# Expert 0's blocks without a fetch of their sums, the last gate on column groups, value loads issued by ScalarE

## The reference

```python
# attention: 8 heads of 64; heads 0-3 see 32 past positions, heads 4-7 every 4th of 128
attn = softmax(where(mask, q @ k.T / 8, -1e9)) ; x = attn @ v          # -> (2304, 512)
h = x @ w_in ; x = (h * cos(h)) @ w_out                                 # 512 -> 2048 -> 512
noisy = x @ w_gate + log1p(exp(x @ w_noise)) * noise                    # 8 experts
top2, top2_w = the two largest of noisy per token, their softmax
for e in range(8):                                                      # 512 -> 1024 -> 512
    for the rows routed to e: out[row] += weight * (relu(x[row] @ w1[e]) @ w2[e])
```

## Time and profile before

| what | us |
|---|---|
| median of three runs | 1009.43 |
| profiled execution, its own time | 1009.55 |
| its span, first to last instruction | 1007.8 |
| TensorE busy | 992.0 (98%) |
| VectorE busy | 575.2 (57%) |
| ScalarE busy | 445.8 (44%) |
| POOL busy | 354.9 (35%) |
| DMA engines, queue of SP | 22.2% of 16 engines |
| granted TensorE clock | 1.00 |

### The profile page before, as it was taken

One profiled execution on the slowest core, in us unless ns is written; L12 is line 12 of the kernel. 1 busy time (PEld: TensorE's weight loads), 2 busy tenths in 40 slices (PEclk: granted clock), 3 DMA queues, 4 the chain that ended last, 5 costly groups with the idle time before them and its releaser, 6 DMA issues. The chain is left out here.

```text
span 1007.8 us, 17738 instructions
## 1 busy us (share of the span) xinstructions
PE 992.0 (98%) x6176; PEld 877.2 (87%) x6176; DVE 575.2 (57%) x1189; ACT 445.8 (44%) x1091; POOL 354.9 (35%) x349
## 2 busy tenths in 40 slices
PE   7999999999999999999999999999999999999998
PEld 5878898888889889889888888999898989999896
DVE  4888766576576576576676754434344444424322
ACT  5989665453454544534547333333132323323111
POOL 2656786222222222222231355143241425133241
PEclk9999999999999999999999999999999999999999
DMA  9787356000000000005006154434353533434130
GB/s 203 178 177 170 74 138 227 33 2 1 31 1 31 0 1 31 1 0 186 14 12 231 55 187 137 144 108 143 130 176 113 177 130 109 142 125 154 41 110 30
DMA packets 101252, 99.60 MB, mean 99 GB/s; under 512 B 72707, under 2 KB 73187, under 8 KB 101184
## 3 DMA queue, kind: packets, MB, share of 16 engines
q1 hardware_dynamic: 86352, 66.38, 22.2%
q0 software_dynamic: 10000, 31.15, 10.0%
q10 hardware_dynamic: 4832, 1.18, 0.7%
HBM read 80.61 MB, written 20.07 MB: 100 GB/s over the span
## 5 line engine op out<-in xcount | busy, mean ns | idle before, releaser
L1807 POOL TENSOR_TENSOR g_lo<-gate,g_hi 128x384 fp32r<-128x384 f32 x95 | 98.0, 1031 | 278.3 <-ACT g_hi L1099 278.3
L1159 ACT ACTIVATE uh_hi<-ps 128x306 fp32r<-128x306 f32 (+1 forms) x112 | 47.8, 426 | 274.1 <-PE ps L155 270.3
L154 PE MATMUL ps<-ux_lo,w_hi 128*128 128x306 f32 (+1 forms) x448 | 136.5, 305 | 0.0
L155 PE MATMUL ps<-ux_hi,w_hi 128*128 128x306 f32 (+1 forms) x448 | 136.0, 304 | 0.0
L153 PE MATMUL ps<-ux_hi,w_lo 128*128 128x306 f32 (+1 forms) x448 | 135.8, 303 | 0.1
L153 PE MATMUL ps<-x_hi,w_lo 128*128 128x384 f32 x384 | 133.6, 348 | 0.1
L1543 DVE SCALAR_TENSOR_TENSOR uh_lo<-ps,uh_hi 128x306 fp32r<-128x306 f32 (+1 forms) x112 | 53.3, 476 | 136.3 <-ACT uh_hi L1159 127.8
L155 PE MATMUL ps<-x_hi,w_hi 128*128 128x384 f32 x384 | 129.3, 337 | 0.0
L154 PE MATMUL ps<-x_lo,w_hi 128*128 128x384 f32 x384 | 129.2, 337 | 0.0
L153 PE MATMUL ps<-w_hi,g_lo 128*128 128x512 f32 x288 | 114.0, 396 | 0.5 <-DVE g_lo L1504 0.5
L155 PE MATMUL ps<-w_hi,g_hi 128*128 128x512 f32 x288 | 114.0, 396 | 0.0
(11 more groups left out here) (230 smaller groups left out, 2033.3 us busy)
## 6 DMA issues: line engine op xcount, KB each, us to landing
xT<-in_w SPq DMA_DIRECT2D x32, 1024.0 KB, 9.2
out<-table SPq DMA_DIRECT2D x18, 256.0 KB, 3.9
y_rows<-y_sb SPq DMA_DIRECT2D x6, 768.0 KB, 3.5
y_sb<-in_w_out SPq DMA_DIRECT2D x16, 256.0 KB, 3.4
q_raw<-in_q SPq DMA_DIRECT2D x40, 96.0 KB, 3.2
k_raw<-in_k SPq DMA_DIRECT2D x30, 96.0 KB, 2.8
w_raw<-in_w_in SPq DMA_DIRECT2D x4, 512.0 KB, 5.0
v_near<-in_v SPq DMA_DIRECT2D x8, 256.0 KB, 3.7
```

Source lines behind the costliest of these rows:

```text
L154: nc.tensor.matmul(psum, s_hi, m_lo, start=False, stop=False)
L155: return nc.tensor.matmul(psum, s_hi, m_hi, start=False, stop=stop)
L1159: nc.scalar.activation(u_h[0][:, f, piece_at[piece]], psH[:, f % 2, 0:PIECE[piece]], ACT.Relu).then_inc(u_hhi, 1)
L1807: nc.gpsimd.tensor_tensor(g2[1][:, f % 2, :], gate[:, f % 2, :], g2[0][:, f % 2, :], ALU.subtract).then_inc(glo_done, 1)
```

## The change

Four things, which can be read apart from each other.

- `acc`, `gather_acc` and their semaphores are gone. `finish(g)` multiplies alone and waits for the scatter of block g-1 in place of the fetch. The early blocks' scatters take their index from where it lies, without a copy, and the first one waits for the zeroed output.
- The last tile's gate is `gate_all`, `copy_turned`, `turn_back`, `copy_all_logits`, as in the loop. The three transposed blocks have three places.
- At the end of the last tile `first_part(0, 1)` on ScalarE goes behind `g_hi` of chunk 15, and `last_low_g` on VectorE goes ahead of all weight parts, `low_x(0)` ahead of `first_part(0, 1)`.
- `load_v(0, 1)` and `load_v(0, 2)` are issued by ScalarE behind `copy_q(0)` and `copy_q(1)` and their keys; `load_w(1)`, `(2)` and `(3)` by ScalarE at the end of steps 3, 6 and 9.

```diff
@@ tiles
-        acc = at(g2_at + 4 * F2, "acc", [P, DM])
+        behind = xT[:].rearrange("p c s -> p (c s)")[:, QUANTA * QW:]
+        yT_end = yT + [behind[:, 0:DM].rearrange("p (d q) -> p d q", q=P)]
+        turned_end = behind[0:GN, DM:DM + P]
@@ SP
-            load_w(0)
-            load_v(0, 1)
+            load_w(sp, 0)
             load_qk(NT)
-            load_v(0, 2)
             for s in range(NT + 1, STEPS + GROUPS):
...
-                if s in (NT + 2, NT + 5, NT + 8):
-                    load_w((s - NT + 1) // 3)
@@ TensorE, behind the last tile
             first_product(0, (1,))
-            gate_y(LAST, 0, 0)
             transpose_x(1)
-            gate_y(LAST, 1, 1)
+            gate_all(LAST)
             transpose_h(0, (0,))
-            gate_y(LAST, 2, 0)
+            turn_back(LAST)
             transpose_h(0, (1,))
@@ ScalarE, tile
-                    if last and f == FC - 1:
-                        first_part(0, 1)
                     act.wait_ge(g_done, m + 1)
...
                     nc.scalar.activation(g2[0][:, f % 2, :], gate[:, f % 2, :], ACT.Copy).then_inc(ghi_done, 1)
-                    if last and f == FC - 2:
-                        first_part(0, 0)
+                    if last and f >= FC - 2:
+                        first_part(0, f - FC + 2)
@@ ScalarE, attention
                 if s < 2:
                     load_rows(act, NT - 2 + s, k, k_raw)
+                    load_v(act, 0, s + 1)
...
+                if s in (3, 6, 9):
+                    load_w(act, s // 3)
@@ ScalarE, behind the last tile
             relu(0, 0)
-            copy_yT(LAST, 0, yT_last[0], yT[0])
-            copy_yT(LAST, 1, yT_last[1], yT[1])
-            copy_logits(LAST, 0)
-            copy_yT(LAST, 2, yT_last[2], yT[0])
+            for b in range(TB):
+                copy_yT(LAST, b, yT_last[b], yT_end[b])
             relu(0, 1)
-            copy_logits(LAST, 1)
             copy_x(1)
-            copy_logits(LAST, 2)
+            copy_turned(LAST)
+            copy_all_logits(LAST)
@@ VectorE, finish
-                dve.wait_ge(acc_in, 16 * (g + 1))
-                nc.vector.scalar_tensor_tensor(out=res[:], in0=eO, scalar=e_all[:, bass.ds(g, 1)], in1=acc[:],
-                                               op0=ALU.mult, op1=ALU.add).then_inc(res_done, 1)
+                if not (isinstance(g, int) and g == 0):
+                    dve.wait_ge(scattered, 16 * g)
+                nc.vector.tensor_scalar(res[:], eO, e_all[:, bass.ds(g, 1)], None, ALU.mult).then_inc(res_done, 1)
@@ VectorE, behind the last tile
+            last_low_g()
             first_part(0, 0)
-            last_low_g()
+            low_x(0)
             first_part(0, 1)
-            low_x(0)
@@ POOL
+            def scatter(g):
+                to = idx_s
+                if isinstance(g, int):
+                    to = slots(1, g)
+                else:
                     pool.wait_ge(scattered, 16 * g)
+                    nc.gpsimd.tensor_copy(idx_s, slots(1, g)).then_inc(iss, 1)
+                    pool.wait_ge(iss, g + 1)
+                if isinstance(g, int) and g == 0:
+                    pool.wait_ge(out_zero, 16 * NB)
                 pool.wait_ge(res_done, g + 1)
...
             gather_x(1)
-            pool.wait_ge(l2_done, FC * NTT)
-            gather_acc(0)
...
                 if g + 2 != EARLY:
-                    scatter(g - 1, g + 2 > EARLY)
+                    scatter(g - 1)
                 if g + 2 > EARLY:
-                    index_acc(g)
                     unit_gather(0, 1, idx_ua, 1)
-                gather_acc(g, g + 2 > EARLY)
-                if g + 2 > EARLY:
                     unit_gather(0, 2, idx_ua, 2)
...
                 scatter(g - 1)
-                gather_acc(g)
             scatter(last)
```

More of the change, by code:

```diff
@@ L393, in load_rows, with load_v, load_w @@
                 eng.dma_start(to[o:o + n, NH:H, :], dilated(src, b)[r, j:j + n, :, :]).then_inc(signal, 16)
+        def load_v(eng, b, g):
+            if b > 0:
+                eng.wait_ge(pv_done, NT * (b - 1) + g + GROUPS + 1)
+            near, p0 = v[b, 0:NH, :, :].rearrange("h (u s) d -> s (h u) d", u=2), WINDOW if g == 0 else 0
+            eng.dma_start(v_near[p0:P, g, :, :, :].rearrange("p h u d -> p (h u) d"),
+                         near[g * TQ - WINDOW + p0:(g + 1) * TQ]).then_inc(v_in_near[g], 16)
+            if g == 0:
+                eng.dma_start(v_near[0:WINDOW, g, :, 1, :],
+                             v[b, 0:NH, S // 2 - WINDOW:S // 2, :].rearrange("h s d -> s h d")
+                             ).then_inc(v_in_near[g], 16)
+            for t in (g, g + GROUPS):
+                for o, r, j, n in segments(t * TQ - WINDOW, TK):
+                    eng.dma_start(v_dil[o:o + n, t, :, :], dilated(v, b)[r, j:j + n, :, :]
+                                 ).then_inc(v_in_dil[t], 16)
+        def load_w(eng, j):
+            if j >= TB:
+                eng.wait_ge(wlo_done, 2 * (j - TB) + 2)
+            d, cols = w_chunk(2 * j)
+            eng.dma_start(w_raw[:, j % TB], w_in_v[:, d, cols.start:cols.start + 2 * WCH]
+                         ).then_inc(w_loaded[j % TB], 16)
         def w_chunk(n):
@@ L463, in _ @@
             sp.sem_inc(d_stored, 16)
[L465 to L479, removed]
             def load_qk(s):
@@ L485, in load_qk @@
                 load_rows(sp, s, k, k_raw)
[L487 to L493, removed]
             def load_ring(at, src):
@@ L697, in transpose_y @@
                 x.then_inc(tp_done, 1)
[L699 to L705, removed]
             def gate_all(i):
                 pe.wait_ge(tp_evac, TB * (i + 1))
+                y = yT_end if isinstance(i, int) and i == LAST else yT_all
                 for d in range(DC):
                     for b in range(TB):
-                        x = nc.tensor.matmul(ps_turned[GQ * b:GQ * (b + 1), :], wgn[:, d, 0:GQ], yT_all[b][:, d, :],
+                        x = nc.tensor.matmul(ps_turned[GQ * b:GQ * (b + 1), :], wgn[:, d, 0:GQ], y[b][:, d, :],
                                              start=(d == 0), stop=(d == DC - 1), skip_group_check=True)
```

40 lines of the change are left out of this document (10 added, 30 removed).

## The result

| | before | after |
|---|---|---|
| median, the two compared | 1010.52 us (1009.1 to 1013.75, 20 runs) | 1012.35 us (1010.84 to 1016.67, 20 runs) |
| profiled execution | 1009.55, span 1007.8 | 1013.62, span 1011.9 |
| ratio after to before | | 1.0023, 95% interval 1.0014 to 1.0032 |

The change costs 2.3 us (1.4 to 3.2). It was forecast at 1008.4 and at most 1011.0. Of the 3.9 us between 1008.4 and 1012.35, 1.1 is not in the change: the forecast started from 1009.43, the median of three runs, and the median of 20 runs of the same kernel is 1010.52. The rest is the change, forecast at -1.05 us and measured at +2.3 by the ratio (+1.8 by the two medians). The profiled execution of after is one of its longer ones, so the two profiles stand 4.1 us apart and not 2.3; the traces are used for where the time is, the ratios for how much it is.

A forecast was written before the change was run, and what follows sets the result against it. TensorE, busy nearly throughout, was taken as the bound. Terms -0.6 - 0.3 - 0.3 + 0.8 + 0.15 - 0.8 = -1.05 us gave 1008.4 us against the 1009.43 median, no change that shows; range 1005.6 to 1011.0 us.

The forecast's parts named there:

- the eight value loads on ScalarE: Between copies of queries 0 and 2: issues delay ScalarE's exponentials and so TensorE, +0.8 us, bounds 0 and 2.7.
- Rival 2: Early loads: ScalarE's and SP's queues share the DMA engines, delay 2.7 us, total +0.85, 1010.3 us; chance 0.10.
- rival 3: Eight value issues: ScalarE blocks on them, +5.4 us, 1014.8; slower from 1.5 us average per issue; chance 0.05.
- Sums: Expert blocks' `finish`: without the fetched sums, TensorE's `h_lo` wait and a later gap shrink, -0.6 and -0.3 us.
- Gate: Last tile: gate grouped on columns takes 2.55 us against 4.15, -1.6 us.
- Order: End of last tile: `g_lo` comes 0.4 us earlier but weight parts come later, cost +1.3 us.
- Weight loads and keys: Query steps: three weight issues on ScalarE cost +0.15 us; SP, relieved, shortens TensorE's key waits, -0.8 us.
- no `acc`: New profile, sign of being right: `acc` appears in no row.
- no `h_lo`: TensorE's waits in the new profile, sign of being right: `h_lo` absent or 0.1 to 0.3 us.
- about 6.7 us at the gate: Sign of being right: first half product's end to block 1's first product takes some 6.7 us instead of 8.3.
- The waits on `xe_lo` and `w_lo`: Between last tile and first half product, sign of being right: TensorE waits 1.3 us or more in all.
- The copy of query 2 past 17 us: ScalarE's early steps: 14 to 16 us would be right; past 17 wrong, pointing to rival 2 or rival 3.

The follow-up runs named there:

- experiment 1: The changed kernel with the two value loads back on SP's queue in their old places: 1007.86 us, ratio 0.997 to the kernel before.
- experiment 5: experiment 2's kernel with eight small DMAs of 16 pieces each added on ScalarE's queue at the value loads' place: 1006.25 us, ratio 0.9986, three runs.
- experiment 6: experiment 2's kernel with the value loads taken off SP and issued by ScalarE later, at the ends of steps 4 and 5: 1006.75 us, ratio 0.9973.
- experiment 4: The changed kernel with 15 products that nothing reads added in three of TensorE's early waits for ScalarE: 1010.49 us, ratio 1.0 to the kernel before.
- experiment 3: The kernel before with only the value loads moved to ScalarE as in the change: 1015.63 us, ratio 1.0049.
- experiment 12: experiment 2's kernel with four products of zeros that nothing reads, ahead of the first queries on TensorE: 1007.97 us, ratio 0.998.
- experiment 2: The changed kernel with value loads back on SP and the old order of ScalarE and VectorE at the last tile: 1006.48 us, ratio 0.9958.

## Why the prediction was wrong

It was wrong in one term of its sum and in one that it didn't have.

- **The term that failed** is the eight value loads on ScalarE: "its issues ran at the low price while all DMA engines were busy, but with few of its own under way; I take the middle, +0.8 us", with bounds 0 and 2.7. The stall was 3.9 us by the trace and 3.0 by the ratios, past the upper bound, and the loads cost 5.4 us in all (experiment 1). The +0.8 is the middle between nothing and 1.6 us, which took SP's prices, 3.22 for four and 2.45 for two; ScalarE paid 4.14 and 3.66. The price belongs to what stands in the queue at that moment, as experiments 5 and 6 show, and rows from another moment are no bound. Rival 2 had the mechanism: issues that can run only so far ahead of the landing, with two queues on the same engines. It put the last issue at 17.1; it ended at 18.3, and its stall of 2.7 us is the nearest to 3.9 in the text. It had 0.10. That it came so near is in part luck: its 362 pieces per us were 427, which makes the issues end earlier, and it left out the pieces of keys that already stood in the queue, about 1080 by the estimate above, which makes them end later. Its 5 us of lead were about 4.1 (1750 pieces unmoved at 18.26).
- **The term that was missing** is TensorE's pace. The text priced a late exponential as a shift of TensorE by as much. But in the profile TensorE not only started late behind its wait, it went on slowly: 2.95 us more by the trace. By the ratios it is 2.3, of which the executions whose clock did not fall have a share that no trace explains (experiment 4). With both, 1.30 us per issue on average made the change slower, where rival 3 asked for 1.5; but slower by 2.3 us, and not by the 3.0 that the text wanted to see. Rival 3 had the sign and 0.05; its argument against itself, SP's 0.95 us on average, was again a row of another moment.
- The rule of the Trainium skill, DMA: Bandwidth & Descriptors, "Issuing engines are not separate DMA queues", that issuing from several engines only saves issue time, usually small beside the transfer, would have made this term zero. The sentence itself is not refuted: 1.30 us of issue on average stand beside 6 to 10 us to landing. What the measurement decides against is to price it at nothing for that: 7.8 us of issue for six DMAs were paid by an engine that computes. The rule of the section "Queues, rings and completion order", engines taking the queues in turn, agrees with the trace as far as 3970 and 3842 packets in nine microseconds do.
- **The others held**, by trace and alone on the chip. Sums: -0.9 forecast, -0.8 by ratio (-1.9 to +0.2); in the profile after -1.3. Gate: -1.6, measured -1.67 and -1.5 (-2.6 to -0.3). Order: +1.3, measured +1.29 and +1.4 (0.4 to 2.4); its chain of starts and ends holds link by link in experiment 1, whose tile stands 0.05 us off that of before: `g_lo` at 530.10, the wait of 0.68 us for `xe_hi`, the half's end at 537.42. Weight loads and keys: -0.65, measured -1.2 with an interval from -2.2 to -0.2, and 0.73 us between query 6 and the last tile. Without the value loads the forecast sum is -1.85; experiment 1 gave -3.0 (-4.3 to -1.7).
- **The parts add up.** Alone they are +0.49, -0.08, -0.15, +0.14 and -0.12 per cent: +0.28, against +0.23 (0.14 to 0.32) together. The five intervals make that sum uncertain by about 0.27 itself, so this says only that nothing large is missing.
- Of the marks that the text named: no `acc`, no `h_lo`, about 6.7 us at the gate (6.59) were right, and the keys' waits did shrink. The waits on `xe_lo` and `w_lo` came in kind and not in size: 1.3 us or more was the mark, 0.5 are listed, and TensorE is idle for 0.69 of the 7.34 us (0.46 of 6.05 before); the rest is in products that follow each other after 1.13 us instead of 0.70. The copy of query 2 past 17 us was the one that said wrong.

## What to carry to other kernels

Before a load is moved to an engine that computes, look at what that engine has in hand where the issue will stand: an issue is hidden behind instructions handed over earlier, and exposed where the engine waits for each one. Price it by rows with as much unmoved in the queue ahead of it, not by a median over the kernel or by a row of another moment. And price a new wait of TensorE of some microseconds twice, once for the wait and once for a slower pace behind it: three profiles here have both (after, experiments 3 and 12), though not every execution does.

## What the hardware showed

- An issue of a DMA on ScalarE's queue lasted 0.47 us with 16 pieces, and for the strided value loads 0.47 to 3.01 us, whatever their own size: 0.47 with 320 pieces, 2.22 with 192, 3.01 and 0.62 with 512. The two longest stood behind some 2000 pieces of their own queue that had not been moved (an estimate from the pieces issued and moved). How many a queue takes before the issuing engine is held no run here tells. SP's queue shows the same (321 to 1957 ns in experiment 2), but nothing computes there.
- TensorE's granted clock was 1.00 or 0.50 in the stretches that lie within one level, 2.4 and 1.2 GHz. In the kernel after it fell in an idle stretch, with 1.14 us of work from 18 to 22 around it, and rose again near 31 us; in experiment 12 it fell behind a wait of 3.88 us and was at 0.50 for some six microseconds.
- The column of the granted clock reads 1.00 from the start of every profile, though in all but experiment 12 the first transposes run at the low pace (0.90 us for four, 0.55 later). There the duration of a known product tells the pace, and the column does not. The Trainium skill, TensorE: Matmul & The Clock Gate, "Part 1: The HAM clock gate", says that the halved rate is where the engine starts and that activity lifts it; these rows agree, and so does experiment 12, whose first transposes were fast after four products more.
- When the pace rises varies from run to run: with the same start, query 3 was slow at 16.81 in the kernel before, and fast at 16.51 in experiment 1 and at 15.16 in experiment 2.
